# A fused recurrence and two expert layers on one core: keys and queries in separate arrays, smaller loads dealt between block copies, and another order of the prologue

## The chip, the cores and the metric

One core of one Trainium2 chip runs the whole program. Its engines are TensorE (PE, matrix products; PEld are its weight loads), VectorE (DVE), ScalarE (ACT), GpSimd (POOL) and SyncE (SP, which here only issues transfers). ACT issues transfers too. The metric is the device time of one execution in microseconds (us), and lower is better.

## The reference, cut to what matters

Three layers follow each other. The first is a recurrence over 768 steps for 4 x 8 heads of size 48; the second sends each of 3072 rows to one of 8 experts; the third puts every row through 4 experts.

```python
for t in range(S):                       # attn: q, k, v (4, 8, 768, 48)
    y[:, :, t] = q_t @ state
    state += beta_t * outer(k_t, v_t - k_t @ state)   # k_t of length one
e = argmax(x @ w_gate)                   # 8 experts, one for each row
x = gate * sigmoid(...) * (relu(x @ w1[e]) @ w2[e])
out = sum_e p[:, e] * (relu(x @ v1[e]) @ v2[e])       # 4 experts
```

## The kernel before

The recurrence is worked in 12 blocks of 64 steps (`NC = 12`). For a block, all heads at once, the kernel needs products of keys with keys (`gram_product`, scaled by ACT into `R`, line L823) and of keys with queries (`query_product`, masked by DVE into `PT`, L1020), and the inverse of a triangular 64x64 matrix for each head. That inverse begins with its 16x16 diagonal pieces: they are copied from `R` to DRAM in 8 small transfers (`gram_blocks<-R`, L293 on SP, L831 on ACT), read back with a piece in each partition (`gram<-gram_blocks`, L300), inverted by DVE (`substitute`, `join_left`, `join_right`), written to DRAM (`inverse_blocks<-inverse`, L305) and copied into `Y` in 8 small transfers (L311, L838 on ACT). `blocks_turned` (DVE, L1068) turns `Y` into `X16`, and PE builds up from 16 to 32 to 64 (`level16_left` to `level32_right`). The inverse is then used by `solve`.

Every engine has its program written out by hand, in its own order, and waits on semaphores. All of this is a pipeline: in round `c` of the main loop, block `c` is solved and its state advanced, block `c+1` gets its levels 16 and 32, the 16x16 pieces of block `c+2` are inverted, and the products of block `c+3` are made. In one round PE works in this order: `predict(c)`, `gram_product(c+3, 0)`, `solve(c)`, `gram_product(c+3, 1)`, `gates_turned`, `advance(c)`, `level16_left(c+1)`, and the rest. The two gram products share one PSUM bank, so the second needs ACT's `gram_scaled(c+3, 0)` to be over.

ACT begins its round with `squares(c+4)` (L809), which reads `kt_sb` (the keys laid out by step, 6 buffers), and only then does `gram_scaled(c+3, 0)`. The squares give the lengths of the keys. The transfers of a round are all issued by SP: two of keys and queries for block `c+4` (`kq_sb`, 5 buffers, one transfer for each half of the partitions), one of `kt_sb` for block `c+5`, one of `vt_sb` for block `c+2`, three that clear a piece of `x_sorted`, and the small copies.

Ahead of the loop stands a prologue that does the same for blocks 0 to 3. It ends for PE with a wait for `const_sb` and `wg`, after which round 0 begins. What follows the loop (routing, and both expert layers) is the same before and after.

Of the kernel before, what the change touches and what calls it, by code (L numbers as in the profile page):

```python
# [5 lines left out]
def fused_kernel(nc, kq, kt, vt, beta, const, gates, w1, w2, probs, v1, v2, out):  # L6
# [12 lines left out]
    NC, _, _, NPAIR, _ = kq.shape  # L19
# [17 lines left out]
    E2 = probs.shape[1]  # L37
# [21 lines left out]
    with ctx:  # L59
# [48 lines left out]
        kq_sb = place("kq_sb", [128, NKQ, NPAIR, 2 * CH])  # L108
# [63 lines left out]
        kq_in = [sem(f"kq_in{i}") for i in range(NKQ)]  # L172
# [13 lines left out]
        gram_out = sem("gram_out")  # L186
# [81 lines left out]
        def _(sp):  # L268
            def load_kq(n, a):
                if n >= NKQ:  # L270
                    sp.wait_ge(read_mm, 2 * (n - NKQ) + 2)
                rows = D if n >= NKQ else CH
                sp.dma_start(kq_sb[HALVES[a]:HALVES[a] + rows, n % NKQ], kq[n, a, 0:rows]).then_inc(kq_in[n % NKQ], 16)

            def load_padding():
                for a in range(2):
                    sp.dma_start(kq_sb[HALVES[a] + D:HALVES[a] + CH, 0], kq[0, a, D:CH]).then_inc(kq_in[0], 16)

            def load_kt(n):
                if n >= NKT:  # L280
                    sp.wait_ge(s_mm, 2 * (n - NKT) + 2)
                sp.dma_start(kt_sb[:, n % NKT], kt[n]).then_inc(kt_in[n % NKT], 16)

            def load_vt(n):
                if n >= NVT:
                    sp.wait_ge(f_mm, 2 * (n - NVT) + 2)
                sp.dma_start(vt_sb[:, n % NVT].rearrange("p h d -> p (h d)"), vt[n]).then_inc(vt_in[n % NVT], 16)

            def blocks_written(n):
                sp.wait_ge(r_ok, 2 * n + 2)  # L290
                for u in range(NU // 2 if n == 0 else 0, NU):
                    rows, cols = slice(BS * u, BS * u + BS), slice(BS * (u % 4), BS * (u % 4) + BS)
                    sp.dma_start(gram_blocks[n % 2, u].rearrange("h j i -> j h i"), R[rows, n % NR, :, cols])\  # L293
                      .then_inc(gram_out, 16)

            def blocks_out(n):
                sp.wait_ge(gram_out, 16 * NU * (n + 1))
# [5 lines left out]
            def blocks_in(n):  # L303
# [10 lines left out]
            load_kt(0)  # L314
            sp.dma_start(beta_sb[:], beta.rearrange("p (c h) -> p c h", h=NPAIR)).then_inc(beta_in, 16)
            sp.wait_ge(kq_in[0], 32)
            load_kt(1)
            blocks_written(0)
            sp.dma_start(const_sb[:], const).then_inc(const_in, 16)
# [10 lines left out]
            load_kt(3)  # L330
            blocks_written(2)
            blocks_out(2)
            load_kq(3, 0)
            load_kq(3, 1)
            load_padding()
            load_kt(4)
            load_vt(1)
            sp.dma_start(wg[:], gates).then_inc(wg_in, 16)
            for half in range(2):
                for p in range(NP):  # L340
                    r0 = (2 * p + half) * S
                    sp.dma_start(p_sb[64 * half:64 * half + 64, p::NP, :],
                                 probs[r0:r0 + S, :].rearrange("(c r) e -> r c e", r=CH)).then_inc(p_in, 16)
            sp.wait_ge(cleared, 2)
            for c in range(NC):
                def clear(i):
                    if c < NC - 1:
                        s0 = 128 * (NZ * c + i)
                        sp.dma_start(x_sorted[s0:s0 + 128, :], zeros[:]).then_inc(zero_out, 16)

                if c + 4 < NC:
                    load_kq(c + 4, 0)
                if c + 3 < NC:
                    blocks_written(c + 3)
                    clear(0)
                    blocks_out(c + 3)
                else:
                    clear(0)
                if c + 4 < NC:
                    load_kq(c + 4, 1)  # L360
                clear(1)
                if c + 5 < NC:
                    load_kt(c + 5)
                if c + 2 < NC:
                    blocks_in(c + 2)
                    load_vt(c + 2)
                clear(2)
# [41 lines left out]
        def _(pool):  # L409
# [16 lines left out]
            def values(n):  # L426
                pool.wait_ge(vt_in[n % NVT], 16 * (n // NVT + 1))
# [73 lines left out]

# [888 lines left out]
```

## Time and profile before

| | us |
|---|---|
| median of 3 runs (lowest, highest) | 1560.58 (1559.11, 1562.19) |
| the profiled execution, its own time | 1574.38 |
| its span, first to last instruction | 1572.6 |
| busy in the span: PE, PEld, DVE, ACT, POOL | 1436.2, 1384.1, 658.9, 292.0, 256.0 |
| mean granted clock of TensorE, as a share of full speed | 0.942 |
| round 0 of the main loop begins on PE at | 83.94 |

Line numbers (L490 and so on) are those of the kernel before. `bank<-kq_sb 64x64` is a gram or query product, `bank<-X,R` a level's left half, `bank<-Y,Z` its right half. In windows "x" counts instructions, and PEclk is the granted clock: 1.00 is 2.4 GHz, 0.5 is 1.2 GHz.

### The profile page before, as it was taken

The page shows a single profiled execution, that of the slowest core. Times are in us where ns is not written, and L with a number is a line of the kernel's source. Part 1 is how long each engine was busy: PE and PEld are TensorE (multiplying, and loading weights), DVE is VectorE, ACT ScalarE, POOL GpSimd, SP SyncE. Part 2 cuts the span into 40 slices and gives each one's busy share as a digit, 9 for nine tenths or more (in the row PEclk, how much of TensorE's full clock was granted, in tenths as well). Part 3 has the DMA queues.
Part 4 walks back from the last instruction along what each step waited for, and adds up shares of the span by engine and source line. Part 5 has one row for each costly group of instructions (what it writes and reads, how often), then busy time and mean ns, then how long its engine had stood idle before and what let it go on. Part 6 is the DMA issues. An engine that isn't in the chain of part 4 may idle for free.

```text
span 1572.6 us, 36732 instructions
## 1 busy us (share of the span) xinstructions
PE 1436.2 (91%) x14818; PEld 1384.1 (88%) x14819; DVE 658.9 (42%) x1301; ACT 292.0 (19%) x631; POOL 256.0 (16%) x132
## 2 busy tenths in 40 slices
PE   4489999996099999997899999999999999999998
PEld 4489889885088888997799999999999999999998
DVE  3457566643255555554343333332233333223332
ACT  2132223212202111100432111111111111111111
POOL 1000101000733354300312202002020020200000
PEclk7689889888599999999799999999999999999999
DMA  5355435322533345111311101001000010000022
GB/s 124 76 114 113 99 85 127 68 72 92 200 115 120 120 135 184 41 40 55 126 46 51 40 0 40 0 0 40 0 28 12 0 40 0 0 0 0 18 52 49
DMA packets 104345, 99.26 MB, mean 63 GB/s; under 512 B 60320, under 2 KB 91424, under 8 KB 102944
## 3 DMA queue, kind: packets, MB, share of 16 engines
q1 hardware_dynamic: 85184, 62.26, 15.7%
q10 hardware_dynamic: 16000, 26.22, 5.2%
q0 software_dynamic: 3072, 9.44, 1.8%
q8 instruction: 75, 1.23, 0.3%
q14 instruction: 14, 0.11, 0.0%
HBM read 72.72 MB, written 25.17 MB: 62 GB/s over the span
## 4 chain that ended last, share of the span: by engine, by line
PE 86%; issue 6%; DMA 3%; DVE 2%; ACT 1%; SPq 1%; ACTq 1%; POOL 0%; DVEq 0%
PE bank L696 23%; PE bank L698 23%; PE bank L697 23%; PE bank L490 11%; PE bank L727 2%; PE bank L601 1%; ACT R L823 1%; PE bank L604 1%; PE bank L620 1%; PE bank L703 1%; DMA wg<-in_gates_dram 1%; SPq L311 0%; PE bank L612 0%; DMA kq_sb<-in_kq_dram 0%; PE bank L759 0%
## 5 line engine op out<-in xcount | busy, mean ns | idle before, releaser
L696 PE MATMUL bank<-x2Th,v1h 128*128 (+1 forms) x768 | 257.8, 336 | 3.6 <-issue 3.6
L696 PE MATMUL bank<-v2h,gTh 128*128 128x384 f32 x768 | 258.3, 336 | 0.0
L698 PE MATMUL bank<-x2Th,v1l 128*128 (+1 forms) x768 | 257.7, 336 | 0.0
L697 PE MATMUL bank<-x2Tl,v1h 128*128 (+1 forms) x768 | 257.7, 335 | 0.0
L698 PE MATMUL bank<-v2h,gTl 128*128 128x384 f32 x768 | 256.6, 334 | 0.0
L697 PE MATMUL bank<-v2l,gTh 128*128 128x384 f32 x768 | 256.6, 334 | 0.0
L1319 DVE SCALAR_TENSOR_TENSOR gTl<-bank,gTh 128x384 fp32r<-128x384 f32 x256 | 142.7, 557 | 271.1 <-ACT gTh L961 271.1
L961 ACT ACTIVATE gTh<-bank 128x384 fp32r<-128x384 f32 x256 | 126.0, 492 | 638.5 <-PE bank L698 630.5
L1328 DVE SCALAR_TENSOR_TENSOR x_all<-bank,p_sb,x_all 128x384 f32 (+1 forms) x192 | 106.7, 611 | 258.9 <-PE bank L698 258.9
L696 PEld LDWEIGHTS bank<-x2Th,v1h 128*128 128x128 f32 x768 | 145.1, 189 | 3.9 <-issue 3.9
L697 PEld LDWEIGHTS bank<-x2Tl,v1h 128*128 128x128 f32 x768 | 145.1, 189 | 0.0
L698 PEld LDWEIGHTS bank<-x2Th,v1l 128*128 128x128 f32 x768 | 145.0, 189 | 0.0
L697 PEld LDWEIGHTS bank<-v2l,gTh 128*128 128x128 f32 x768 | 144.2, 188 | 0.0
L696 PEld LDWEIGHTS bank<-v2h,gTh 128*128 128x128 f32 x768 | 144.2, 188 | 0.0
L698 PEld LDWEIGHTS bank<-v2h,gTl 128*128 128x128 f32 x768 | 144.1, 188 | 0.0
L490 PE MATMUL bank<-kq_sb 64*64 64x64 f32 (+1 forms) x1536 | 65.3, 245 | 37.1 <-DMA kq_sb<-in_kq_dram 14.4
L490 PEld LDWEIGHTS bank<-kq_sb 64*64 64x64 f32 (+1 forms) x1536 | 59.6, 158 | 39.2 <-DMA kq_sb<-in_kq_dram 14.8
L696 PE MATMUL bank<-w2h,hTh 128*128 x248 | 86.4, 348 | 2.5 <-DVE hTl L1281 2.5
L475 POOL CAST v1h<-v_raw 128x1536 fp32r<-128x1536 f32 x7 | 10.3, 1473 | 478.2 <-PE bank L698 478.2
L698 PE MATMUL bank<-w2h,hTl 128*128 x248 | 84.0, 339 | 0.0
L697 PE MATMUL bank<-w2l,hTh 128*128 x248 | 83.8, 338 | 0.0
L696 PE MATMUL bank<-w1h,xsTh 128*128 x186 | 76.7, 412 | 7.5 <-issue 4.8
(167 smaller groups left out, 1960.6 us busy)
## 6 DMA issues: line engine op xcount, KB each, us to landing
w_raw<-in_moe_w_dram ACTq DMA_DIRECT2D x16, 1536.0 KB, 6.9
v_raw<-in_moe_w_dram SPq DMA_DIRECT2D x16, 768.0 KB, 4.5
x_sorted<-zeros SPq DMA_DIRECT2D x33, 192.0 KB, 3.9
xs_in<-x_sorted SPq DMA_DIRECT2D x33, 192.0 KB, 2.3
y_sorted<-y_sb SPq DMA_DIRECT2D x31, 192.0 KB, 1.9
kq_sb<-in_kq_dram SPq DMA_DIRECT2D x14, 384.0 KB, 5.6
kt_sb<-in_kt_dram SPq DMA_DIRECT2D x12, 392.0 KB, 5.7
vt_sb<-in_vt_dram SPq DMA_DIRECT2D x12, 384.0 KB, 4.1
```

The source lines that it names most:

```text
L490: return pe.matmul(dst, lhsT, rhs, start=True, stop=True)
L601: pe.matmul(bank[5 + p][half_rows(a), small(p, h)], kq_sb[half_rows(a), c % NKQ, h, CH:2 * CH], state[half_rows(a), c % 2, h], start=True, ...
L604: last = pe.matmul(bank[5 + p][half_rows(a), small(p, h)], PT[half_rows(a), c % NPT, h], delta[half_rows(a), h], start=(c == 0), stop=True)
L620: last = pe.matmul(bank[7][0:2 * NE, 0:NP * 128], wg[:, m, :], xT_gate[:, m].rearrange("q p n -> q (p n)"), start=(m == 0), stop=(m == KD ...
L696: pe.matmul(dst, lh, rh, start=first, stop=False)
L697: pe.matmul(dst, lh, rl, start=False, stop=False)
L698: return pe.matmul(dst, ll, rh, start=False, stop=last)
L703: ins = pe.transpose(bank[5][:, 128 * m:128 * m + 128], xs_in[:, 128 * m:128 * m + 128], ident)
L727: ins = pe.transpose(bank[2 + half][:, 128 * m:128 * m + 128], h_sb[:, k0:k0 + 128], ident)
L961: act.activation(gTh[:, f, :], bank[f][:, 0:BN], ACT.Relu).then_inc(g_hi, 1)
L1319: dve.scalar_tensor_tensor(out=gTl[:, f, :], in0=bank[f][:, 0:BN], scalar=0.0, in1=gTh[:, f, :].bitcast(f32), op0=ALU.max, op1=ALU.subtract)\
L1328: dve.scalar_tensor_tensor(out=a, in0=bank[4 + t][:, 0:DM], scalar=p_sb[:, bass.ds(tile, 1), bass.ds(e, 1)].rearrange("p o d -> p (o d)"), ...
```

## The change

Keys and queries come as two arrays (`kq_sb` is `[128, 5, 2, 16, 64]`), with two transfers each and semaphores of their own, `k_in` and `q_in`. `kt_sb` and `vt_sb` are loaded as two transfers of 64 partitions. The loads and the clearing of `x_sorted` are no longer issued ahead of or behind the 8 small copies but between them (`beside_gram`, `beside_inverse`). In the prologue the transfers and a few steps of PE, DVE and ACT stand in another order; the four transfers of `probs` become one, and there is a `gram_out` semaphore for each of two buffers.

```diff
-            def load_kq(n, a):
+            def load_k(n, a):
                 if n >= NKQ:
                     sp.wait_ge(read_mm, 2 * (n - NKQ) + 2)
                 rows = D if n >= NKQ else CH
-                sp.dma_start(kq_sb[HALVES[a]:HALVES[a] + rows, n % NKQ], kq[n, a, 0:rows]).then_inc(kq_in[n % NKQ], 16)
+                sp.dma_start(kq_sb[HALVES[a]:HALVES[a] + rows, n % NKQ, 0], kq[n, a, 0, 0:rows]).then_inc(k_in[n % NKQ], 16)
...
+            def beside_gram(c, u):
+                if c + 4 < NC:
+                    if u == 1:
+                        load_k(c + 4, 0)
+                    if u == 3:
+                        load_k(c + 4, 1)
+                    if u == 5:
+                        load_q(c + 4, 0)
+                    if u == 7:
+                        load_q(c + 4, 1)
+                if u == 6:
+                    clear(c, 0)
+
+            def beside_inverse(c, u):
+                if c + 5 < NC:
+                    if u == 1:
+                        load_kt(c + 5, 0)
+                    if u == 3:
+                        load_kt(c + 5, 1)
+                if c + 2 < NC:
+                    if u == 5:
+                        load_vt(c + 2, 0)
+                    if u == 7:
+                        load_vt(c + 2, 1)
+                if u == 2:
+                    clear(c, 1)
+                if u == 6:
+                    clear(c, 2)
...
-            load_kq(1, 0)
-            load_kq(1, 1)
-            load_kt(2)
-            load_vt(0)
+            load_kt(2, 0)
+            load_kt(2, 1)
+            load_q(1, 0)
+            load_q(1, 1)
+            blocks_out(1)
             blocks_in(0)
-            load_kq(2, 0)
-            blocks_out(1)
-            load_kq(2, 1)
+            load_k(2, 0)
+            load_k(2, 1)
+            load_vt(0, 0)
+            load_vt(0, 1)
+            sp.dma_start(wg[:], gates).then_inc(wg_in, 16)
+            load_q(2, 0)
+            load_q(2, 1)
             blocks_in(1)
...
@@ block.tensor: prologue
             gram_product(0, 0)
             gram_product(0, 1)
+            gram_product(1, 0)
             query_product(0, 0)
-            gram_product(1, 0)
             gram_product(1, 1)
+            query_product(0, 1)
             pe.wait_ge(inverse_out, 16)
-            keep_warm(16)
-            query_product(0, 1)
+            keep_warm(14)
             level16_left(0)
@@ block.scalar: prologue
             for a in range(2):
-                act.dma_start(kq_sb[HALVES[a]:HALVES[a] + D, 0], kq[0, a, 0:D]).then_inc(kq_in[0], 16)
+                act.dma_start(kq_sb[HALVES[a]:HALVES[a] + D, 0, 0], kq[0, a, 0, 0:D]).then_inc(k_in[0], 16)
+            for a in range(2):
+                act.dma_start(kq_sb[HALVES[a]:HALVES[a] + CH, 1, 0], kq[1, a, 0]).then_inc(k_in[1], 16)
+            for a in range(2):
+                act.dma_start(kq_sb[HALVES[a]:HALVES[a] + D, 0, 1], kq[0, a, 1, 0:D]).then_inc(q_in[0], 16)
...
             blocks_written(1)
-            first_in()
             squares(2)
             root(2)
+            first_in()
@@ block.vector: prologue
             join_right(0)
-            dve.wait_ge(const_in, 16)
-            query_masked(0, 0)
             squares_summed(2)
+            query_masked(0, 1)
             key_lengths(2)
-            blocks_turned(0)
-            query_masked(0, 1)
             for i in range(1, HB):
                 substitute(1, i)
+            blocks_turned(0)
+            join_left(1)
             query_masked(1, 0)
+            join_right(1)
             level16_taken(0)
-            join_left(1)
-            join_right(1)
             query_masked(1, 1)
```

On SP, at the end of the prologue, the transfers stand so before (from the `Y` copies of block 1 on):

```order
L311 DMA Y<-inverse_blocks 16x16x16 x8
L282 DMA kt_sb<-in_kt_dram 128x784
L293 DMA gram_blocks<-R 16x16x16 x8
L300 DMA gram<-gram_blocks 128x256
L273 DMA kq_sb<-in_kq_dram 64x2048 x2
L277 DMA kq_sb<-in_kq_dram 16x2048 x2
L282 DMA kt_sb<-in_kt_dram 128x784
L287 DMA vt_sb<-in_vt_dram 128x768
L338 DMA wg<-in_gates_dram 128x48
L342 DMA p_sb<-in_moe_domain_probs_dram 64x12x4 x4
```

and so in the change, from the same place (L292 is `kt_sb`, L298 `vt_sb`, L338 and L347 the copies from `R` and the reading back; `wg` stands 5 rows further up, outside of this piece):

```order
L292 DMA kt_sb<-in_kt_dram 64x784 x2
L338 DMA gram_blocks<-R 16x16x16 x8
L274 DMA kq_sb<-in_kq_dram 64x1024 x2
L347 DMA gram<-gram_blocks 128x256
L280 DMA kq_sb<-in_kq_dram 64x1024 x2
L298 DMA vt_sb<-in_vt_dram 64x768 x2
L285 DMA kq_sb<-in_kq_dram 16x1024
L286 DMA kq_sb<-in_kq_dram 16x1024
L285 DMA kq_sb<-in_kq_dram 16x1024
L286 DMA kq_sb<-in_kq_dram 16x1024
L292 DMA kt_sb<-in_kt_dram 64x784 x2
L398 DMA p_sb<-in_moe_domain_probs_dram 128x96
```

The wait for `wg` moved away from the end, and `kt_sb` of block 4 now has the loads of `vt_sb` and four pieces of padding ahead of it.

In a round of the main loop SP issues this before, from the reading back of the pieces to the end of the round:

```order
L300 DMA gram<-gram_blocks 128x256
L273 DMA kq_sb<-in_kq_dram 48x2048
L349 DMA x_sorted<-zeros 128x384
L282 DMA kt_sb<-in_kt_dram 128x784
L305 DMA inverse_blocks<-inverse 128x256
L311 DMA Y<-inverse_blocks 16x16x16 x8
L287 DMA vt_sb<-in_vt_dram 128x768
L349 DMA x_sorted<-zeros 128x384
```

and this in the change:

```order
L352 DMA inverse_blocks<-inverse 128x256
L358 DMA Y<-inverse_blocks 16x16x16 x2
L292 DMA kt_sb<-in_kt_dram 64x784
L358 DMA Y<-inverse_blocks 16x16x16
L303 DMA x_sorted<-zeros 128x384
L358 DMA Y<-inverse_blocks 16x16x16
L292 DMA kt_sb<-in_kt_dram 64x784
L358 DMA Y<-inverse_blocks 16x16x16 x2
L298 DMA vt_sb<-in_vt_dram 64x768
L358 DMA Y<-inverse_blocks 16x16x16
L303 DMA x_sorted<-zeros 128x384
L358 DMA Y<-inverse_blocks 16x16x16
```

`kt_sb` of block `c+5` moved from ahead of the writing of the inverse to behind it, its second half behind four copies of `Y`.

On ACT the middle of the prologue stands so before (L831 are the copies from `R` of block 1, L838 those into `Y` of block 0, L809 and L814 are `squares(2)` and `root(2)`):

```order
L823 ACTIVATE R<-bank,minus_gain 128x64 x16
L831 DMA gram_blocks<-R 16x16x16 x8
L838 DMA Y<-inverse_blocks 16x16x16 x4
L809 ACTIVATE k_sq<-kt_sb 128x768
L814 ACTIVATE norms<-norms 128x16
```

and so in the change:

```order
L871 ACTIVATE R<-bank,minus_gain 128x64 x16
L879 DMA gram_blocks<-R 16x16x16 x8
L857 ACTIVATE k_sq<-kt_sb 128x768
L862 ACTIVATE norms<-norms 128x16
L886 DMA Y<-inverse_blocks 16x16x16 x4
```

The squares and the root of block 2 moved ahead of the copies into `Y`.

## Rows read from the trace of the kernel before

**Rows 1.** Windows: prologue, then rounds from one first `delta` product to the next.

```profile
0.00:83.94 83.94, 38.25 (x704) 37.08 (x706) 31.27 (x89) 17.54 (x53) 8.08 (x20) 0.67 0.50 104
...
109.52:133.32 23.80, 23.63 (x726) 22.28 (x722) 17.55 (x42) 7.78 (x28) 2.36 (x2) 1.00 0.57 117
...
157.58:189.58 32.00, 29.78 (x725) 27.31 (x723) 16.86 (x41) 7.66 (x28) 2.37 (x2) 0.79 0.46 104
189.58:221.33 31.75, 29.09 (x726) 27.27 (x723) 16.78 (x42) 7.67 (x28) 4.73 (x4) 0.84 0.45 103
...
269.00:299.47 30.47, 28.62 (x726) 27.05 (x723) 16.70 (x42) 7.24 (x28) 3.78 (x4) 0.83 0.46 99
```

**Rows 2.** Timeline of the prologue, all engines: start, length, engine, what, idle before.

```profile
19.27 0.17 DVE L1010 TENSOR_SCALAR minus_gain<-gain 128x16 f32<-128x16 f32 x1
...
25.07 1.97 PE L490 MATMUL bank<-kq_sb 64*64 64x64 f32 x32 [11.20 <-DMA kq_sb<-in_kq_dram]
...
32.88 5.15 ACTq L831 DMA_DIRECT2D gram_blocks<-R  x8
...
39.42 0.34 SPq L300 DMA_DIRECT2D gram<-gram_blocks  x1
...
45.54 3.63 PE L490 MATMUL bank<-X,R 64*64 64x32 f32 x64 [9.00 <-DVE X L1068]
...
59.39 0.34 SPq L305 DMA_DIRECT2D inverse_blocks<-inverse  x1
...
61.10 4.24 SPq L311 DMA_DIRECT2D Y<-inverse_blocks  x8
...
65.39 0.45 SPq L282 DMA_DIRECT2D kt_sb<-in_kt_dram  x1
...
71.14 0.34 SPq L300 DMA_DIRECT2D gram<-gram_blocks  x1
...
74.04 1.98 PE L490 MATMUL bank<-kq_sb 64*64 64x64 f32 x32 [11.29 <-DVE PT L1020]
...
82.18 0.84 ACT L809 ACTIVATE k_sq<-kt_sb 128x768 f32<-128x768 f32 x1 [11.43 <-DMA kt_sb<-in_kt_dram]
...
83.94 1.97 PE L490 MATMUL bank<-kq_sb 64*64 64x64 f32 x32 [7.93 <-DMA wg<-in_gates_dram]
...
88.14 1.12 PE L490 MATMUL bank<-kq_sb 64*64 64x64 f32 x32
```

**Rows 3.** Timeline of PE, in the round of 157.58.

```profile
165.97 1.28 PE L490 MATMUL bank<-X,R 64*64 64x32 f32 x20 [2.06 <-issue]
```

**Rows 4.** DMA queues (packets, MB, share of 16 engines) in 160:163, then 163:167.

```profile
q1 hardware_dynamic: 406, 0.83, 93.3%
q14 instruction: 1, 0.01, 1.6%
...
q8 instruction: 1, 0.02, 2.2%
```

**Rows 5.** Timelines of ACT and SP in one round of the main loop.

```profile
111.84 1.75 ACT L823 ACTIVATE R<-bank,minus_gain 128x64 f32<-128x64 f32 x8 [1.41 <-PE bank L490]
...
127.39 0.85 ACT L809 ACTIVATE k_sq<-kt_sb 128x768 f32<-128x768 f32 x1 [0.28 <-DMA kt_sb<-in_kt_dram]
132.48 1.74 ACT L823 ACTIVATE R<-bank,minus_gain 128x64 f32<-128x64 f32 x8 [4.25 <-PE bank L490]
```

```profile
124.90 0.32 SPq L305 DMA_DIRECT2D inverse_blocks<-inverse  x1
128.35 4.97 SPq L311 DMA_DIRECT2D Y<-inverse_blocks  x8
```

**Rows 6.** Tile views of kt_sb, kq_sb, and x_sorted (84:350): issue to landing, SP's transfers.

```profile
DMA to landing us min/median/max: 3.0/5.7/8.4
...
DMA to landing us min/median/max: 4.6/5.6/8.1
...
DMA to landing us min/median/max: 2.0/3.9/5.8
```

More of the change, by code:

```diff
@@ L36, in fused_kernel @@
     F = w1.shape[2]
-    E2 = probs.shape[1]
+    E2 = probs.shape[2]
     N = NB * S
@@ L171, in fused_kernel @@
         wg_in = sem("wg_in")
-        kq_in = [sem(f"kq_in{i}") for i in range(NKQ)]
+        k_in = [sem(f"k_in{i}") for i in range(NKQ)]
+        q_in = [sem(f"q_in{i}") for i in range(NKQ)]
         kt_in = [sem(f"kt_in{i}") for i in range(NKT)]
@@ L185, in fused_kernel @@
         pt_ok = sem("pt_ok")
-        gram_out = sem("gram_out")
+        gram_out = [sem(f"gram_out{i}") for i in range(2)]
         gram_in = [sem(f"gram_in{i}") for i in range(2)]
@@ L281, in load_kt, with load_vt @@
                     sp.wait_ge(s_mm, 2 * (n - NKT) + 2)
-                sp.dma_start(kt_sb[:, n % NKT], kt[n]).then_inc(kt_in[n % NKT], 16)
-            def load_vt(n):
+                rows = slice(HALVES[a], HALVES[a] + CH)
+                sp.dma_start(kt_sb[rows, n % NKT], kt[n, rows]).then_inc(kt_in[n % NKT], 16)
+            def load_vt(n, a):
                 if n >= NVT:
                     sp.wait_ge(f_mm, 2 * (n - NVT) + 2)
-                sp.dma_start(vt_sb[:, n % NVT].rearrange("p h d -> p (h d)"), vt[n]).then_inc(vt_in[n % NVT], 16)
@@ L289, in blocks_written, with clear @@
-            def blocks_written(n):
+                rows = slice(HALVES[a], HALVES[a] + CH)
+                sp.dma_start(vt_sb[rows, n % NVT].rearrange("p h d -> p (h d)"), vt[n, rows]).then_inc(vt_in[n % NVT], 16)
+            def clear(c, i):
+                if c < NC - 1:
+                    s0 = 128 * (NZ * c + i)
+                    sp.dma_start(x_sorted[s0:s0 + 128, :], zeros[:]).then_inc(zero_out, 16)
+            def beside_gram(c, u):
[10 more added lines that the diff above has]
+                    clear(c, 0)
@@ L290, in blocks_written @@
+            def blocks_written(n, c=None):
                 sp.wait_ge(r_ok, 2 * n + 2)
@@ L312, in blocks_in @@
                       .then_inc(y0_in[n % NY], 16)
-            load_kt(0)
+                    if c is not None:
+                        beside_inverse(c, u)
+            load_kt(0, 0)
+            load_kt(0, 1)
             sp.dma_start(beta_sb[:], beta.rearrange("p (c h) -> p c h", h=NPAIR)).then_inc(beta_in, 16)
-            sp.wait_ge(kq_in[0], 32)
-            load_kt(1)
+            load_kt(1, 0)
+            load_kt(1, 1)
+            sp.dma_start(const_sb[:], const).then_inc(const_in, 16)
@@ L335, in _ @@
+            load_vt(1, 0)
+            load_vt(1, 1)
             load_padding()
[L336 to L343, printed above, removed]
+            load_kt(4, 0)
@@ L356, in _ @@
                     blocks_out(c + 3)
                 else:
[L358 to L363, printed above, removed]
+                    for u in range(NU):
+                        beside_gram(c, u)
                 if c + 2 < NC:
-                    blocks_in(c + 2)
-                    load_vt(c + 2)
-                clear(2)
+                    blocks_in(c + 2, c)
+                else:
+                    for u in range(NU):
+                        beside_inverse(c, u)
@@ L500, in keep_warm, with loads_of @@
                     mul(bank[7][:, 0:128], ones[:], ones[:])
+            def loads_of(n):
+                return 32 * (n // NKQ + 1) + (32 if n >= NKQ and n % NKQ == 0 else 0)
             def key_rows(n):
@@ L567, in predict @@
                     for a in HALVES:
-                        last = mul(bank[3 + p][half_rows(a), small(p, h)], kq_sb[half_rows(a), c % NKQ, h, 0:CH],
+                        last = mul(bank[3 + p][half_rows(a), small(p, h)], kq_sb[half_rows(a), c % NKQ, 0, h],
                                    state[half_rows(a), c % 2, h])
@@ L1115, in _ @@
             key_lengths(1)
+            dve.wait_ge(const_in, 16)
+            query_masked(0, 0)
             dve.wait_ge(eye_ok, 1)
```

71 lines of the change are left out of this document (40 added, 31 removed).

## The prediction

> **What bounds the kernel now.** I read the windows first, then the timeline of the prologue, then what PE waits for in the loop. What lies behind the recurrence is not touched, so only its first 380 us count. In the windows [rows 1] the reader is to see two kinds of loss. The prologue takes 83.94 us, in which PE is busy for 38.25. The rounds that follow take 23.80 us when nothing goes wrong (PE busy 23.63, clock 1.00), but 32.00, 31.75 and 30.47 in three of them, with a clock of 0.79 to 0.84. These three are 22.8 us over 3 x 23.80.
>
> The prologue is a chain of waits [rows 2]. PE's first product of block 1 waits 11.20 us for the keys and queries. The chain goes on through ACT's 8 copies (32.88), the reading back (39.42), the first level (45.54, after 9.00 us of waiting), the inverse of block 1 (59.39), 8 copies, then the load of `kt_sb` for block 3 (65.39), whose squares, lengths and masks PE awaits at 74.04 (11.29 us). Last, PE waits 7.93 us for `wg`, which is issued behind every other load.
>
> The long rounds begin with an idle time that no engine and no transfer explains: 2.06 us of "issue" in the middle of one group of products [rows 3]. The transfers tell why [rows 4]: from 160 to 163 the data queue fills 93.3% of the 16 engines and of PE's instruction queue (q8) there is no packet; one comes in the next stretch, 163 to 167. PE had run out of instructions. The granted clock of that round is 0.79, so part of it ran at 1.2 GHz instead of 2.4. The fetch costs more through the clock than by itself.
>
> **The change part by part.** The sum is made against the profiled execution's own time, 1574.38 (span 1572.6, 1.8 us outside of it). That is 13.8 over the median of the runs, 1560.58.
>
> Prologue, first part. The keys of block 1 are loaded by ACT at the start. Their product can then run when block 0's is scaled, long before 19.27 + 0.17 = 19.4, when the scale of block 1 is known. From there: 1.75 to scale the first half, 1.97 for the second product, 1.75 to scale it, together 24.9; hand-overs make it 25.1, where row 32.88 stands now. The 8 copies take 5.15: 30.3, and as now (38.03 to 39.42) 1.4 later they have landed. SP now reads back block 1 first and only then writes block 0's inverse, at 32.0. This is a new wait: block 0's inverse is ready some 5 us earlier. 1.7 us for it to land (59.39 to 61.10), 1.9 for four copies on ACT, up to 2.3 for the last to land: 37.9; turning it is about 1.3. So the first level starts at about 39.3, not 45.54: 6.2 us less.
>
> Second part. From there to the inverse of block 1 it is 59.39 - 45.54 = 13.85 us now. DVE no longer does `level16_taken` and its transpose between `query_masked(1, 0)` and the joins, and `join_left` moves into the time of PE's first level. I work it out as X ready, 3.63 for the level, 1.97 for a query product, 0.7 for its mask and 1.75 for `join_right`: 8.0. That puts the write at 47.3, 12.1 us less than now. Whatever PE gains by a higher clock there comes on top.
>
> Third part. The 8 copies, `kt_sb` of block 3 and the masks follow as now, so the last query product ends at 76.0 - 12.1 + 0.3 = 64.2 (0.3 for the load in halves), and the 7.93 us for `wg` are gone. But another load is late then. `kt_sb` of block 4 is issued behind `vt_sb`, padding and queries; now the loads that begin behind the reading back at 71.14 bring it in at 82.18, so 11 us. With `vt_sb` ahead of it I put 12, and they begin at about 58: it is in at about 70. ACT does `squares(4)` ahead of `gram_scaled(3, 0)`, so this lands in PE's `gram_product(3, 1)`: 70 + 0.84 + 1.74 = 72.6, against 88.14 now [rows 2]. So the prologue gives 15 us and not 22. Bounds: 10, if the transfers that now start together at the beginning delay `kt_sb` of block 0 and the copies, and 18, if block 4's keys come sooner. I take 15.
>
> Instruction fetch. The loads of a round now come in two bursts, around 960 KB issued within 2 us each. They will be issued one by one between small copies, some 0.5 us each, so in 5 to 6 us. The data queue should then not be full for 3 us on end. If no fetch is late, the three long rounds become 23.8, 22.8 us less in the profile. The runs without a profile are 13.8 us faster than the profiled one, and I do not know where; if all of that is fewer late fetches, only 9 of the 22.8 are left to gain there. I take 12 for the median.
>
> The page "Runtime: NRT & Kernel Launch" of the Trainium skill, under "Instruction fetch mechanics", says that instructions come in blocks of 16 KiB on a queue of the sequencer's own, and that crossing into the next is "mostly hidden". By that rule this term would be nothing, and the sum 12 higher. The 2.06 us of [rows 3] speak against it here.
>
> The new wait. `kt_sb` of block c+5 was issued before the inverse was written and now comes behind it. I count from the end of ACT's second scaling, 111.84 + 1.75 = 113.6 [rows 5]. The inverse is written at +11.3. With no load in the queue it lands in 1.7, as at 59.39, instead of 3.45. The copies begin at +13.0, at 0.45 to 0.5 each; the second half of `kt_sb` is the seventh transfer, so it is issued at +15.9. ACT needs it there in time for `squares` (0.85) ahead of `gram_scaled` at 132.48, which is +18.9: by +18.0. It has 2.1 us. The nearest rows [rows 6] are 2.0 for the fastest clearing of 192 KB and 3.0 for the fastest whole `kt_sb` of 392 KB. So it is late by 0 to 0.9 us. On top of that, 8 small copies take 4.97 us in this round and 4.24 in [rows 2], where 8 at 0.5 would take 3.9: somewhere in most groups of copies about a us is lost, and more often than not it will fall ahead of the load. I take 1.0 us late in each of the 7 rounds that have such a load. PE then waits in front of `gram_product(c+3, 1)`, where it has no slack, and everything is behind it: 7 us. The clock fell in the round of the 2.06 us wait [rows 3]; I reckon that it falls in two of the seven. A long round cost 22.8 / 3 = 7.6, of which the waits are some 2 to 3, so a fall is put at 4.5, two at 9 us. Together 16 us. Bounds: 0 (always in time) and 43 (every round 1.4 late, and every one with a fall of the clock: 7 x 6.1).
>
> At nothing go: the copies from `R` (a whole round of slack), `probs` in one transfer (SP has no hurry then), the loads of keys and queries (issued a round ahead), the copies into `Y`: they now carry five loads among them, but begin 1.7 us sooner.
>
> Sum in the profile: 1574.4 - 15 - 23 + 16 = 1552. For the median: 1560.6 - 15 - 12 + 16 = 1549.6. I say 1549.
>
> **The rivals.**
>
> - Forecast, 0.45: as above, 1541 to 1557.
> - `kt_sb` comes in time. For it: the fastest 192 KB landed in 2.0 us. Against it: the us that groups of copies lose. 1560.6 - 15 - 12 = 1533. Chance 0.2.
> - Fetches are late as before. For it: the bytes are the same, and in the second group of copies the loads are as dense as PE will ever see them. Then 1560.6 - 15 + 16 = 1562, no change. Chance 0.18.
> - Slower: every load of `kt_sb` is late by more than a us, and the clock falls every time. A load of half the partitions may run at half the speed: the fastest 512 KB of keys and queries into 64 partitions took 4.6 us, a whole `kt_sb` of 392 KB into 128 took 3.0 [rows 6]. Two halves would then take about 0.9 us more than one whole. It decides from a landing later than +19 on. 1560.6 - 15 - 12 + 43 = 1576. Chance 0.17. "DMA: Bandwidth & Descriptors" in the Trainium skill ("Rules for kernel authors") advises against two transfers to disjoint halves of the partitions: they serialize, and one of 128 partitions should be used. By that rule the change is on this side; [rows 6] agree.
>
> **How the numbers follow.** A measurement of this kernel can tell about 0.2%, 3 us, from no change. Faster: the forecast, the second case and a little of the third: 0.70. Same: most of what is left around 1562: 0.10. Slower: the fourth and the rest: 0.20. The forecast's own range is 1541 to 1557; cases of both signs together ask for 1531 to 1570.
>
> **What would show it.** In the profile after: round 0's `gram_product(3, 1)` at about 72.6; ACT's `squares` in the rounds with "DMA kt_sb" as what ended its wait, and PE waiting about a us for `R` behind `solve`; no "issue" of a us or more on PE between 90 and 370; rounds of about 24.8. I am wrong if the copies at the very start land late, if the clock falls with each wait for `R`, or if the profile after has long rounds begun by "issue".

## The result: 0.5% slower, and the profile after

| | before | after |
|---|---|---|
| median of 20 runs each, us | 1561.97 | 1571.18 |
| lowest, highest | 1552.63, 1579.84 | 1564.01, 1579.07 |
| the profiled execution | 1574.38 | 1574.62 |

The ratio is 1.0052, with a 95% interval of 1.0028 to 1.0075. The prediction was 1549 with a range of 1531 to 1570 and a chance of 0.70 for faster. It had the wrong sign, and the time is just outside the range. The two profiled executions agree, but that of before lies 12 us above its median and that of after 3 us, so rounds of the two profiles must not be subtracted as if both were typical.

New line numbers: a product of PE is L534 (it was L490), `squares` L857, `gram_scaled` L871, `blocks_turned` L1120, `load_kt` L292, the copies into `Y` L358.

The windows of after, cut where DVE's first `delta` (L1151) of a round starts, as the rounds of [rows 1] are. (Only the first row there ends elsewhere: at 83.94, where round 0 begins on PE, 3.48 us ahead of its first `delta`.) The columns are length, busy time of PE, PEld, DVE, ACT and POOL, then clock, DMA share and GB/s.

```profile
0.00:69.59 69.59, 38.27 (x770) 36.96 (x773) 31.97 (x89) 16.69 (x52) 7.62 (x19) 0.73 0.59 119
69.59:99.03 29.44, 22.45 (x648) 22.23 (x647) 16.89 (x41) 6.45 (x22) 1.47 (x1) 0.83 0.40 96
99.03:127.19 28.16, 25.05 (x726) 23.50 (x724) 16.88 (x41) 7.74 (x27) 2.36 (x2) 0.94 0.45 101
127.19:153.93 26.74, 25.09 (x726) 23.59 (x724) 16.89 (x41) 7.59 (x26) 2.37 (x2) 0.94 0.44 105
...
239.53:266.81 27.28, 25.05 (x726) 23.53 (x724) 16.88 (x41) 7.66 (x26) 2.36 (x2) 0.94 0.41 98
```

Before had rounds of 23.80 and some of 30 to 32. After has none of either kind in rounds 1 to 7: all take 26.7 to 30.5, at a clock of 0.94, one at 0.89. The end of the recurrence shows the sum: the first product behind it (`gate_small`, of the routing) starts at 385.42, and at 383.10 before.

The prologue is as short as forecast. The timeline of after, PE, ACT and SP taken together in order of time:

```profile
40.69 2.06 PE L534 MATMUL bank<-X,R 64*64 64x32 f32 x64 [0.20 <-DVE X L1120]
...
47.17 0.34 SPq L352 DMA_DIRECT2D inverse_blocks<-inverse  x1
...
64.20 3.68 PE L534 MATMUL bank<-kq_sb 64*64 64x64 f32 x64 [9.52 <-DVE PT L1072]
...
73.26 0.84 ACT L857 ACTIVATE k_sq<-kt_sb 128x768 f32<-128x768 f32 x1 [12.43 <-DMA kt_sb<-in_kt_dram]
...
75.88 1.97 PE L534 MATMUL bank<-kq_sb 64*64 64x64 f32 x32 [5.33 <-ACT R L871]
```

These answer to the rows at 45.54, 59.39, 74.04, 82.18 and 88.14 of [rows 2]. The last is `gram_product(3, 1)`: 12.3 us sooner.

The loop loses. Of the view of waits in 90:360 of after three lines matter (in all us, times, longest):

```profile
ACT k_sq L857 <- DMA kt_sb<-in_kt_dram: 51.6, 7, 9.0
...
DVE X L1120 <- DMA Y<-inverse_blocks: 23.4, 10, 3.9
...
PE bank L534 <- ACT R L871: 19.5, 8, 4.5
```

ACT's wait for `kt_sb` is no loss by itself, since ACT has time to spare. What it passes on is: PE waits for `R` once in each of rounds 1 to 7, for 3.11, 1.65, 2.38, 4.48, 2.24, 2.23 and 3.23 us, together 19.3. One such round, first SP, then ACT, then PE:

```profile
118.42 0.34 SPq L352 DMA_DIRECT2D inverse_blocks<-inverse  x1
120.61 0.82 SPq L358 DMA_DIRECT2D Y<-inverse_blocks  x2
121.47 0.47 SPq L292 DMA_DIRECT2D kt_sb<-in_kt_dram  x1
121.98 0.58 SPq L358 DMA_DIRECT2D Y<-inverse_blocks  x1
122.61 0.45 SPq L303 DMA_DIRECT2D x_sorted<-zeros  x1
123.10 0.43 SPq L358 DMA_DIRECT2D Y<-inverse_blocks  x1
123.58 0.49 SPq L292 DMA_DIRECT2D kt_sb<-in_kt_dram  x1
```

```profile
104.60 1.75 ACT L871 ACTIVATE R<-bank,minus_gain 128x64 f32<-128x64 f32 x8 [1.71 <-PE bank L534]
...
127.12 0.84 ACT L857 ACTIVATE k_sq<-kt_sb 128x768 f32<-128x768 f32 x1 [6.13 <-DMA kt_sb<-in_kt_dram]
127.86 1.73 ACT L871 ACTIVATE R<-bank,minus_gain 128x64 f32<-128x64 f32 x8
```

```profile
129.74 1.15 PE L534 MATMUL bank<-kq_sb 64*64 64x64 f32 x32 [1.65 <-ACT R L871]
```

From the end of the second scaling (104.60 + 1.75 = 106.35) the inverse is written at +12.1 (forecast +11.3), the second half of `kt_sb` issued at +17.2 (+15.9) and landed at +20.8 (+17.9 to +18.9). By the round of before it was needed at +18.0; in after PE comes a little later itself, and 20.8 - 1.65 says that +19.1 would have been soon enough. Over rounds 0 to 6, which load for rounds 1 to 7, the means are +12.2, +18.1 and +21.9.

### The profile page after: what moved, and what is told of

It reads as the page before. It is cut to its first block, busy times and chain, and to the rows that moved or that the text cites. A ratio compares the mean times of both kernels' runs of the same rounds, so it can differ in the third digit from the quotient of the medians.

```text
span 1572.8 us, 36797 instructions
## 1 busy us (share of the span) xinstructions
PE 1432.8 (91%) x14814; PEld 1380.6 (88%) x14815; DVE 658.6 (42%) x1301; ACT 291.1 (19%) x631; POOL 255.9 (16%) x132
## 4 chain that ended last, share of the span: by engine, by line
PE 80%; issue 7%; DMA 5%; SPq 3%; DVE 2%; ACT 2%; ACTq 0%; POOL 0%; DVEq 0%
PE bank L744 23%; PE bank L746 23%; PE bank L745 22%; PE bank L534 7%; DMA kt_sb<-in_kt_dram 3%; PE bank L775 2%; ACT R L871 1%; SPq L358 1%; DMA inverse_blocks<-inverse 1%; PE bank L649 1%; PE bank L652 1%; PE bank L660 1%; PE bank L751 1%; SPq L303 0%; DMA gram_blocks<-R 0%
## 5 line engine op out<-in xcount | busy, mean ns | idle before, releaser
L534 PE MATMUL bank<-kq_sb 64*64 64x64 f32 (+1 forms) x1536 | 62.2, 240 | 45.6 <-ACT R L871 35.8
L534 PEld LDWEIGHTS bank<-kq_sb 64*64 64x64 f32 (+1 forms) x1536 | 56.7, 153 | 46.9 <-issue 46.6
```

The source lines that it names most:

```text
L534: return pe.matmul(dst, lhsT, rhs, start=True, stop=True)
```

## The experiments

Each ratio is of the kernel to the kernel before on the same chip, with its 95% interval. The theories, as the expectations name them: K, the landing of `kt_sb` sets the loop; Y, the late copies into `Y` do, because `blocks_turned` waits for them and PE's first level for it; H, two half transfers cost more than one whole; F, late instruction fetches come from what is queued beside them.

**The prologue alone.** The loop's transfers go back to the bursts and places of before, in halves and with keys and queries apart; the prologue stays as after. (The edit is shown without its conditions on `c`.)

```diff
 for c in range(NC):
+    load_k(c + 4, 0); load_q(c + 4, 0)
     blocks_written(c + 3)
+    clear(c, 0)
     blocks_out(c + 3)
+    load_k(c + 4, 1); load_q(c + 4, 1); clear(c, 1)
+    load_kt(c + 5, 0); load_kt(c + 5, 1)
     blocks_in(c + 2)
+    load_vt(c + 2, 0); load_vt(c + 2, 1); clear(c, 2)
-    beside_gram(c, u)
...
-    beside_inverse(c, u)
```

> The changed kernel with the loads of the main loop issued in the two bursts of the kernel before, ahead of and behind the small copies (still in halves and with keys and queries apart). This leaves the prologue as the change. If the prologue's gain is real in the timed runs: 12 to 15 us under the kernel before, about 1548, with the odd long round begun by an idle time of issue on PE. If the prologue gives nothing in the end (its gain lost in the rounds behind it): about 1562.

Measured: 0.9896 (0.9859 to 0.9934), 1548.27 against 1564.42, so 16 us gained.

**The loop alone.** The loop of after behind the order of before's prologue on all engines:

```diff
-            blocks_out(1)
-            blocks_in(0)
-            load_k(2, 0)
-            load_k(2, 1)
+            blocks_in(0)
+            load_k(2, 0)
+            load_q(2, 0)
+            blocks_out(1)
...
-            gram_product(1, 0)
             query_product(0, 0)
+            gram_product(1, 0)
```

> The changed main loop behind the prologue order of the kernel before (SP, PE, ACT and DVE; keys and queries apart, probs in one transfer). If the two parts add up: the changed kernel plus the 12 to 15 us of the prologue, about 1583, with a wait for R of 1.5 to 4.5 us in seven rounds. If the loads of the new prologue are what makes the loop late, the seven waits shrink and it is near 1562.

Measured: 1.0163 (1.0123 to 1.0203), 1587.12, so 25 us lost by the ratio, 19 to 32 by its interval. PE's seven waits for `R` are 2.1 to 3.5 us, together 19.0. The parts add up: -16 + 25 = +9, each of them to some 6 us, and the whole change is 1.0052, +8. Nothing says that prologue and loop hinder each other.

**`kt_sb` early.** After, with both halves issued behind the reading back of the pieces and ahead of the writing of the inverse, where before had its whole load:

```diff
                     blocks_out(c + 3)
+                if c + 5 < NC:
+                    load_kt(c + 5, 0)
+                    load_kt(c + 5, 1)
...
-                    if u == 1:
-                        load_kt(c + 5, 0)
-                    if u == 3:
-                        load_kt(c + 5, 1)
```

> The changed kernel with one edit: both halves of kt_sb for block c+5 are issued right behind the reading back of the pieces, ahead of the writing of the inverse, and no longer between the copies into Y. Theory K (the late kt_sb is what costs): PE's waits for R in front of the second gram product, 19.3 us in the seven rounds of the changed kernel, go to under 0.3 each, the clock stays at 1.00 in those rounds, a round takes about 24; the time is some 30 us under the changed kernel, about 1540 where the kernel before has 1562. Rival Y (the copies into Y are late too and take its place): PE then waits for X16 in front of the first level, 1 to 2 us a round, and the time is 1550 to 1556.

Measured: 0.9966 (0.9937 to 0.9995), 1560.58. The waits for `R` in the loop are gone (the longest is 0.2 us), as K says. But the time is 20 us above what K expected. The timelines of DVE and PE in this kernel say where it went:

```profile
129.69 1.25 DVE L1118 STREAM_TRANSPOSE X<-Y 128x1024 f32<-128x1024 f32 x1 [3.80 <-DMA Y<-inverse_blocks]
131.04 2.23 PE L532 MATMUL bank<-X,R 64*64 64x32 f32 x64 [1.64 <-issue]
...
257.05 1.25 DVE L1118 STREAM_TRANSPOSE X<-Y 128x1024 f32<-128x1024 f32 x1 [5.46 <-DMA Y<-inverse_blocks]
...
258.39 3.11 PE L532 MATMUL bank<-X,R 64*64 64x32 f32 x64 [3.30 <-issue]
```

The profile puts PE's idle times down to "issue", and they look like those of [rows 3]. They are something else. In [rows 3] PE stops inside a group, with 20 of its 64 products still to come, where it waits for no semaphore. Here all 64 products of `level16_left` come behind the idle time, and that step waits for `X16`, the result of `blocks_turned` (the DVE rows). They start 0.10 and 0.09 us after DVE ends (129.69 + 1.25 = 130.94, 257.05 + 1.25 = 258.30), and DVE had waited 3.80 and 5.46 us for the copies into `Y`. So this is rival Y: once `kt_sb` is out of the way, the late copies into `Y` take its place. In four of rounds 1 to 7 PE waits so, for 1.64, 0.74, 0.96 and 3.30 us. The time is above Y's range too (1550 to 1556).

Its rounds are now 23.7, 27.1, 23.8, 24.7, 26.4, 23.7 and 30.3: good ones and long ones, as in [rows 1], but the long ones have another cause.

**Seven buffers.** The other way to take the wait away: every transfer stays where after has it, but `kt_sb` has a seventh buffer and is loaded a round sooner.

```diff
-NKQ, NKT, NVT, NR, NPT, NY = 5, 6, 3, 3, 4, 3
+NKQ, NKT, NVT, NR, NPT, NY = 5, 7, 3, 3, 4, 3
...
-                        load_kt(c + 5, 0)
+                        load_kt(c + 6, 0)
```

> The changed kernel with a seventh buffer of kt_sb: at the same two places among the copies into Y it now loads block c+6, a round ahead, and the prologue loads block 5 too. SP's order in the loop and the halves stay as in the changed kernel. Theory K (the landing of kt_sb is what costs): no wait for R over 0.3 us in the rounds, and most of the 25 us that the loop's order costs come back: a ratio to before of about 0.990. Rival Y (the copies into Y land at +24 and take its place in front of the first level): PE waits there 1 to 2 us a round instead, and the ratio stays at 0.998 or over.

Measured: 0.9917 (0.989 to 0.9943), 1556.72, some 21 us under after. No wait for `R` in the loop is over 0.2 us. Six idle times of "issue" of 1.0 us or more stand in the loop, and each is again a wait for `X16`: all 64 products of the first level start 0.10 us after the end of `blocks_turned`. The longest, with the DMA queues in 204:211 and 211:212 (packets, MB, share of 16 engines):

```profile
205.25 2.07 PE L536 MATMUL bank<-delta,kt_sb 64*64 64x48 f32 x64
...
208.76 1.25 DVE L1122 STREAM_TRANSPOSE X<-Y 128x1024 f32<-128x1024 f32 x1 [4.96 <-DMA Y<-inverse_blocks]
...
210.11 3.63 PE L536 MATMUL bank<-X,R 64*64 64x32 f32 x64 [2.79 <-issue]
```

```profile
q1 hardware_dynamic: 2223, 0.91, 59.7%
...
q8 instruction: 1, 0.02, 10.2%
```

The 64 `delta` products are complete ahead of the stop, and PE goes on at 210.11, ahead of the next packet of its instruction queue (q8, in 211:212). So it had its instructions and lacked `X16`. The ratio lies at K's expectation (0.990), the waits are Y's: both are right in part. In the prologue, where this kernel loads block 5 as well, PE waits 7.13 us for `R` and not 5.33.

What dealing the loads out does to late fetches can be read from all fourteen traces, if only idle times of "issue" inside a group of products are counted, from 60 to 385 us. The seven kernels that issue the loads of a round in bursts (before and six of the experiments) have one to five of 1 us or more each, the longest 2.71. The seven that deal them out (after and six of the experiments) have none: the longest is 0.82, in after 0.48. That is one profiled execution of each. In after and in two of the others PE also waits 1.65 us or more for `R` in each of rounds 1 to 7, in which its queue could fill (not shown); but in `kt_sb` early and here there are rounds of 23.7 with no such wait, and no late fetch either.

**`kt_sb` later.** The dose the other way: `vt_sb` and `kt_sb` change places among the copies.

```diff
                 if c + 5 < NC:
-                    if u == 1:
+                    if u == 5:
                         load_kt(c + 5, 0)
-                    if u == 3:
+                    if u == 7:
                         load_kt(c + 5, 1)
```

> The changed kernel with the halves of kt_sb and of vt_sb changed in place among the copies into Y: vt_sb behind the second and fourth copy, kt_sb behind the sixth and eighth. Theory K: kt_sb is issued 4 transfers (2 to 2.5 us) later, PE's wait for R grows by that much in each of seven rounds, the time grows by 14 to 20 us: a ratio to before of about 1.016. Rival (the wait is set by something else, or the queue drains all the same): 1.005 as the changed kernel.

Measured: 1.0266 (1.024 to 1.0291), 1609.58, so 33 us more than after. `kt_sb` is issued at +21.9 to +23.9 and landed at +25.1 to +27.0. The seven waits for `R` are 6.5 to 7.5 us, together 48.2, 28.9 more than in after. The direction is K's. The size was above the expectation, because the second half goes out behind seven more transfers (four copies, both halves of `vt_sb` and a clear) and not four, 4.7 us later in the mean and not 2 to 2.5. One row of ACT and one of PE in this kernel:

```profile
137.01 0.84 ACT L857 ACTIVATE k_sq<-kt_sb 128x768 f32<-128x768 f32 x1 [11.35 <-DMA kt_sb<-in_kt_dram]
```

```profile
139.63 1.65 PE L534 MATMUL bank<-kq_sb 64*64 64x64 f32 x26 [6.87 <-ACT R L871]
```

**`kt_sb` whole.** After, with one transfer of 128 partitions at the place of the first half:

```diff
-                rows = slice(HALVES[a], HALVES[a] + CH)
-                sp.dma_start(kt_sb[rows, n % NKT], kt[n, rows]).then_inc(kt_in[n % NKT], 16)
+                if a == 0:
+                    sp.dma_start(kt_sb[:, n % NKT], kt[n]).then_inc(kt_in[n % NKT], 16)
```

> The changed kernel with kt_sb loaded by one transfer of 128 partitions, in the loop at the place of the first half, in the prologue as well. Theory K with the halves as its cause: the one transfer lands like a half does, about +18.5 us from the end of the second scaling instead of +20.7 to +24.0, the wait for R shrinks to under 0.7 a round, the time is about 1548 to 1552. Theory K with the place as its cause: what stands ahead of it (inverse, two copies) is the same, so the wait shrinks only by what the second issue came later, and PE still waits about 1 us a round with falls of the clock: 1556 to 1562.

Measured: 0.9896 (0.9857 to 0.9936), 1547.80: 24 us under after, for one line. Issued at +15.8 in the mean, where the last half of after goes out at +18.1, the whole load lands at +19.8 instead of +21.9: 392 KB in one transfer take 4.1 us, the last 196 KB alone 3.8. So nearly all of it is the place in SP's row of transfers. The time is what the expectation had for the halves as the cause, the landing (+19.8, not +18.5) and the waits are nearer to the place as the cause. The waits for `R` sum to 9.1 us instead of 19.3, and in the prologue `gram_product(3, 1)` starts at 72.64. The rounds are still 24.4 to 27.4 us, but the seven are only 12.5 over 7 x 23.80, where those of after are 30.2 over. The clock falls in two of the seven, behind waits of 1.77 and 2.36 us, and not behind those of 1.35 and 2.67.

**Halves in the kernel before.** Both loads as two halves, at the places of before:

```diff
-                sp.dma_start(kt_sb[:, n % NKT], kt[n]).then_inc(kt_in[n % NKT], 16)
+                for a in HALVES:
+                    sp.dma_start(kt_sb[a:a + CH, n % NKT], kt[n, a:a + CH]).then_inc(kt_in[n % NKT], 16)
```

> The kernel before with one edit: kt_sb and vt_sb by two transfers of 64 partitions each, at the places of the one. Theory H: the loads hold the DMA engines longer, more fetches of instructions are late, the time is 3 to 10 us over the kernel before. Rival: no difference (within 0.2%).

Measured: 0.9976 (0.9947 to 1.0004). Two transfers of half the partitions cost nothing that can be measured where PE does not wait for them, so H as a price in itself falls.

**Whole loads in bursts.** The kernel with the prologue alone, and `kt_sb` and `vt_sb` whole everywhere (the edit of `kt_sb` whole, and the same for `vt_sb`).

> The prologue's order of the change, the loop's loads in the two bursts of the kernel before, and kt_sb and vt_sb again in one transfer of 128 partitions everywhere. Theory H (halves cost DMA time by themselves): faster than the same kernel with halves (ratio to before 0.9896) by 3 to 10 us, so a ratio of about 0.985. Rival (halves cost nothing where their landing is not waited for): 0.9896 again.

Measured: 0.9847 (0.9798 to 0.9896), 1546.47. The interval overlaps that of the prologue alone, so whether whole loads gain in bursts stays open. What difference there is stands in the prologue: `gram_product(3, 1)` starts at 69.91, and at 76.81 in the kernel with halves. One wait is left there:

```profile
69.91 1.97 PE L546 MATMUL bank<-kq_sb 64*64 64x64 f32 x32 [4.13 <-ACT R L883]
```

**`kt_sb` of block 4 sooner.** That wait is for `squares(4)`. The same kernel, with this load moved ahead of the reading back of block 2:

```diff
+            load_kt(4, 0)
             blocks_out(2)
             load_q(3, 0)
...
             load_padding()
-            load_kt(4, 0)
-            load_kt(4, 1)
```

> The kernel e5_bursts_whole with the load of kt_sb for block 4 issued ahead of the reading back of block 2's pieces, and no longer behind queries, vt_sb and padding. If PE's wait of 5 to 6 us for R in round 0 is from that load, it goes to under 1 us, the clock need not fall there, and the time is 5 to 10 us under e5_bursts_whole, about 1538. If another load takes its place (the reading back, or the queries of block 3), it is within 2 us of e5_bursts_whole.

Measured: 0.9805 (0.9767 to 0.9843), 1537.39, 9 us under the kernel without the move on the same chip; the intervals overlap, the profiled executions are 1536.79 and 1549.93. PE no longer waits for `R` there, but in the middle of the `delta` products that follow it stops for 2.71 us, with 37 of 64 still to come (no q8 packet in 64:67, one in 67:68):

```profile
70.38 1.25 PE L545 MATMUL bank<-delta,kt_sb 64*64 64x48 f32 x37 [2.71 <-issue]
```

Its rounds 1 to 3, in windows:

```profile
90.75:115.36 24.61, 23.87 (x726) 22.37 (x724) 16.90 (x42) 7.70 (x28) 2.37 (x2) 1.00 0.49 113
115.36:139.36 24.00, 23.75 (x726) 22.27 (x722) 16.88 (x41) 7.78 (x28) 2.36 (x2) 1.00 0.54 116
139.36:163.25 23.89, 23.72 (x726) 22.34 (x723) 16.89 (x42) 7.69 (x28) 2.37 (x2) 1.00 0.49 117
```

**Idle products ahead of the wait.** After, with 8 products of `ones` ahead of `gram_product(c+3, 1)` in rounds 1 to 7, into a bank that is free there (extra work, nothing left out):

```diff
+                if 1 <= c < 8:
+                    for _ in range(8):
+                        mul(bank[1][:, 0:128], ones[:], ones[:])
                 if ahead:
                     gram_product(c + 3, 1)
```

> The changed kernel with 8 idle products of 128x128 (into a bank that nobody reads then) ahead of PE's wait for the second gram product in rounds 1 to 7. They fill about 2 us of a wait of 2 to 4.5 us. If the fall of the clock behind each wait (3.41 us at half speed in each of seven rounds) is a cost of its own, the clock stays at 1.00 there and the time is 7 to 12 us under the changed kernel (ratio about 0.998). If the landing of kt_sb alone sets the round, it stays within 3 us of the changed kernel (1.005).

Measured: 1.0019 (0.9991 to 1.0047), 1567.80. The clock now holds through the loop but for one stretch. Windows of this kernel:

```profile
93.52:158.37 64.85, 59.06 (x1691) 55.97 (x1691) 36.69 (x87) 17.84 (x61) 4.73 (x4) 1.00 0.44 104
158.37:161.78 3.41, 3.41 (x42) 2.96 (x43) 2.08 (x2) 1.45 (x8) 1.87 (x2) 0.50 0.14 51
161.78:294.90 133.12, 128.64 (x3749) 121.29 (x3750) 84.30 (x207) 38.81 (x133) 11.71 (x11) 1.00 0.45 103
```

In after the clock falls to 1.2 GHz behind each of the seven waits, six times for 3.41 us and once for 6.83. Taking away all but one gains 0.33%, 5 us, with intervals that touch: between the two expectations. That is less than the falls cost. The seven rounds of after take 196.8 us, 30.2 over 7 x 23.80; 19.3 of that are waits, which leaves 10.9 for the falls. In this kernel the seven rounds take 187.9, 8.9 less, though the idle products cost some 1.7 us in a round that had no wait left (25.45). But in round 8, which has no idle products, PE now waits 2.26 us for `X16` and the round takes 28.6 instead of 22.9.

**The clears last, twice.** The clearing of `x_sorted` is 192 KB in each of 33 transfers. In the kernel before, and in the one with `kt_sb` of block 4 sooner, all 33 are moved to rounds 8 to 10, so that the rounds of the prediction carry 576 KB less each.

```diff
-                    if c < NC - 1:
-                        s0 = 128 * (NZ * c + i)
+                    if 8 <= c < NC - 1:
+                        s0 = 128 * (11 * (c - 8) + i)
...
-                clear(2)
+                for i in range(11):
+                    clear(i)
```

> The kernel before with one edit: the 33 transfers of 192 KB that clear x_sorted are issued in rounds 8 to 10, 11 in each, and no longer 3 in each round from 0 on. Theory F (full data queues make fetches of PE's instructions late): rounds 0 to 7 move 576 KB less each, fewer of them are begun long by an idle time of issue, the time is 5 to 15 us under the kernel before (ratio 0.990 to 0.997). Rival (the fetches are late for another reason): ratio 1.000, or above it, if the 11 transfers at a round's end delay what follows.

> e7_kt4_sooner (ratio 0.9805: the prologue's order of the change, bursts, whole kt_sb and vt_sb, kt_sb of block 4 sooner) with the clearing of x_sorted in rounds 8 to 10. Theory F: the last short waits of issue in its rounds go, rounds of 23.8, 0 to 5 us under e7: ratio 0.978 to 0.980. Rival: the transfers at the end delay the routing that waits for them, and it is slower than e7.

Measured: 0.996 (0.994 to 0.9979) for the first, with idle times of "issue" of 1.3 to 1.9 us inside groups still in its rounds, and 0.9801 (0.9777 to 0.9824) for the second, the same as 0.9805 without the move. Fewer bytes beside the fetches help a little or not at all: by the first ratio F in this form is worth 0.4%, by the second nothing. The loads are still issued in bursts in both. With all the bytes but no bursts there was no such idle time, so the bursts and not the sum of bytes go with it.

The kernel with `kt_sb` of block 4 sooner, with and without its clears last, is 2% under before and 2.5% under after: 1537 us.

## Why the prediction was wrong, step by step

- **Prologue, -15: right.** The first level starts at 40.69 (39.3 forecast), the inverse is written at 47.17 (47.3), the last query product starts at 64.20, the time given for its end. `kt_sb` of block 4 lands in time for squares at 73.26, against 70, and `gram_product(3, 1)` starts at 75.88, against 72.6. The profile gives 12.3 us, the timed runs of the prologue alone 16, both inside the bounds of 10 to 18. The load that was named as late next was the right one; with whole loads, taking it away gives some 9 more (intervals that overlap).
- **The new wait, "7 us": the right mechanism, and the step that failed, by its size.** The wait is in all seven rounds, at the place given, but for 2.76 us and not 1.0: 19.3 us together. Four terms make it, as means over rounds 0 to 6. The inverse is written 0.9 later than forecast; DVE works in order, and `blocks_turned` ahead of it waits for the late copies into `Y` (23.4 us in 10 times), which I take for the cause. The write takes 2.2 to the first copy and not 1.7. The six transfers ahead of the second half take 3.7 and not 2.9. And the landing took 3.8, between 3.5 and 4.5. The prediction had taken 2.0 to 3.0, the fastest of [rows 6], while the medians in the same rows were 3.9 and 5.7; it argued that the queue would be empty, but the first half and a clear go ahead of the second. Landed at +21.9 instead of about +19 is the failed number.
- **"On top of that" the clock, 9 us: near the measured 10.9 by luck.** It fell behind all seven waits and not two, but for 3.41 us at a time (once 6.83), at about 1.6 us a fall and not 4.5. Waits and falls together are the 30.2 us by which rounds 1 to 7 of after exceed 7 x 23.80, where 16 was forecast. The 14 more take the forecast of 1549.6 to 1564. The loop alone measured +25 for everything in it, where 16 - 12 = +4 was forecast.
- **Instruction fetch, -12: as far as the traces reach the mechanism came true, the size is not measured.** It said that with loads issued between copies no fetch would be late. After has no idle time of a us inside a group, nor has any other kernel with the loads dealt out. The 12 us are probably too many. Rounds 1 to 7 of before are 23.4 us over 7 x 23.80 in the profile, but those of the six experiments with bursts are only 2.2 to 12.8 over, and the median of before lies 12 under its profiled execution.
- **The copies into `Y` at nothing: wrong, though mostly hidden in after.** They have five loads and clears among them and land late. In after PE waits for `R` first, and `X16` is ready meanwhile; in rounds 9 and 10, where that wait is gone, it waits 1.18 and 0.57 us for `X16`. Without the waits for `R` (`kt_sb` early, seven buffers) the waits for `X16` sum to 6.6 and 7.0 us in rounds 1 to 7, and these rounds are still 13.1 and 14.8 us over 7 x 23.80, with falls of the clock in three of the seven each. That is why the two cures gave 13 and 21 us and not 30. Round 8 to the end of the recurrence takes 89.6 us in after's profile and 83.6 in before's; only part of these 6 us is explained by these two waits and the falls of the clock near them.
- **The sum again,** as an estimate: -15 for the prologue, -12 for the fetches, +30 for rounds 1 to 7, +6 for the rounds behind them make +9, and the medians differ by 9.2. Since the -12 are not measured by themselves, that it comes out so near is partly luck. The time lies between the third rival (1562) and the fourth (1576). The traces show the fourth: every load of `kt_sb` late by more than a us, and a fall of the clock each time, at 30 us and not 43. (The 43 take 6.1 a round, where 1.4 + 4.5 are 5.9; nothing hangs on it.)
- The page "Runtime: NRT & Kernel Launch" of the Trainium skill ("Instruction fetch mechanics") calls the crossing into a new block "mostly hidden". In the kernels with bursts idle times up to 2.71 us inside a group speak against it, so it was right to doubt the rule.
- **The halves at nothing:** in the kernel before they measure 0.9976 (0.9947 to 1.0004), so as a price in itself that was right. In after one whole transfer, in the loop and in the prologue, is worth 24 us, because it is issued 2.3 us sooner than the second half was.
- **The profiled execution of before** was 12 us over the median of its runs, and its three long rounds were read as what before always does. The prediction cut the 22.8 us to 12 for that. The 20 runs of before spread from 1552.63 to 1579.84, and I take it (not shown) that the lower ones have few long rounds. The clock fits that: of 23 runs of before on one chip the four fastest have a mean granted clock of 0.950 or 0.951, the four slowest of 0.942 to 0.944.

**What stays open.** What the late fetches cost in the median, and why they come with the bursts when fewer bytes do not help. That they are fetches is read from the place of the idle times inside a group and from the q8 packets and was not tried by itself; a kernel with shorter instruction streams was not run. Nor was a kernel that deals out the loads but has `kt_sb` and the copies into `Y` both in time.

## What to carry to other kernels

When a load moves behind a round trip through DRAM, write down when it was needed, when it will be issued and when it will land, and take the landing from the median of rows with the same neighbours in the queue, not from the fastest row. A load that is awaited should be one transfer, placed ahead of the small copies; each transfer and copy ahead of it costs half a us, and now and then one or two more. A load that is put between small copies delays the copies as well, so ask who waits for them, even if another wait hides it today. When the profile says "issue", look whether the engine stopped inside a group or at its first instruction, and in the second case compare the time with the end of every step that it waits for: here waits for `X16` of up to 3.30 us stand in the profile as "issue". And look at how the profiled execution stands to the other runs before counting its worst rounds as a gain.

## What the runs showed of the hardware

- Behind waits of 1.65 to 4.5 us on PE in a loop that is otherwise busy the clock fell for 3.41 us, once for 6.83 (after); behind one of 2.67 us it did not fall (`kt_sb` whole).
- SP needs 0.42 to 0.50 us to issue most of the loads and copies of after, but in most groups one takes a us or more. SP in the round shown, of after; both rows are in the way of loads:

```profile
111.06 1.44 SPq L303 DMA_DIRECT2D x_sorted<-zeros  x1
...
124.12 1.90 SPq L358 DMA_DIRECT2D Y<-inverse_blocks  x2
```

- Among others in the queue a transfer of about 192 KB takes over 3 us. The DMA issues on the profile page of after (KB each, median us to landing), in the whole run:

```profile
kq_sb<-in_kq_dram SPq DMA_DIRECT2D x28, 192.0 KB, 3.2
kt_sb<-in_kt_dram SPq DMA_DIRECT2D x24, 196.0 KB, 3.6
vt_sb<-in_vt_dram SPq DMA_DIRECT2D x24, 192.0 KB, 3.3
```
